# Attention's first stretch: where the scores of the block three later stand in a step of TensorE

## The reference, cut to what matters

```python
def _attn_ref(q, k, v, tau):
    scale = 1.0 / np.sqrt(q.shape[-1])
    scores = scale * np.matmul(q, k.transpose(0, 1, 3, 2))
    thresh = np.max(scores, axis=-1, keepdims=True) - tau
    scores = np.where(scores >= thresh, scores, -1000000000.0)
    scores = scores - np.max(scores, axis=-1, keepdims=True)
    attn = np.exp(scores)
    attn = attn / (np.sum(attn, axis=-1, keepdims=True) + 1e-09)
    return np.matmul(attn, v).astype(np.float32)
```

## Time and profile before

| | |
|---|---|
| Median of three runs | 1185.02 us (1183.88 to 1187.9) |
| The profiled execution's own time | 1193.75 us |
| Its span, from the first to the last instruction | 1192.0 us |
| PE busy | 1093.7 us, 92% of the span |
| DVE, ACT, POOL busy | 593.7, 439.3 and 347.3 us |
| Mean granted clock of PE | 0.953 |
| Last copy of a turned block in the first stretch ends | 112.8 us after the span's start |

### The profile page before, as it was taken

One profiled execution on the slowest core, in us unless ns is written; L12 is line 12 of the kernel. 1 busy time (PEld: TensorE's weight loads), 2 busy tenths in 40 slices (PEclk: granted clock), 3 DMA queues, 4 the chain that ended last, 5 costly groups with the idle time before them and its releaser, 6 DMA issues. The chain is left out here.

```text
span 1192.0 us, 20141 instructions
## 1 busy us (share of the span) xinstructions
PE 1093.7 (92%) x7130; PEld 956.7 (80%) x7131; DVE 593.7 (50%) x1164; ACT 439.3 (37%) x730; POOL 347.3 (29%) x324
## 2 busy tenths in 40 slices
PE   6889899999989999998999989899947999999995
PEld 5566699898979989887998987799946887887784
DVE  4565555656455565645556552222257344255641
ACT  5465443333354333335333332211144244144530
POOL 4454005433411452341235314055011121121111
PEclk9898999999999999989999988999957999999998
DMA  6776115335161452415134112022057335154501
GB/s 152 177 188 156 30 27 140 96 94 141 53 152 42 125 130 81 120 60 145 41 105 113 69 36 94 18 72 71 1 198 267 123 123 186 37 189 143 206 32 37
DMA packets 110650, 127.28 MB, mean 107 GB/s; under 512 B 67213, under 2 KB 67213, under 8 KB 110544
## 3 DMA queue, kind: packets, MB, share of 16 engines
q1 hardware_dynamic: 104480, 114.54, 33.9%
q0 software_dynamic: 3520, 10.75, 2.8%
q10 hardware_dynamic: 2544, 0.59, 0.2%
HBM read 87.90 MB, written 10.22 MB: 82 GB/s over the span
## 5 line engine op out<-in xcount | busy, mean ns | idle before, releaser
L753 ACT ACTIVATE ex<-score_banks,stat 128x576 f32<-128x576 f32 x132 | 97.8, 741 | 199.6 <-DVE stat L857 199.6
L657 PE MATMUL mlp_banks<-u_hi,w_hi 128*128 128x320 f32 (+1 forms) x512 | 159.2, 311 | 12.4 <-DVE hid_lo L916 9.5
L665 PE MATMUL mlp_banks<-hid_hi,w_hi 128*128 128x320 f32 (+1 forms) x512 | 158.7, 310 | 7.6 <-DVE z L924 7.2
L462 POOL TENSOR_TENSOR w_lo<-stage,w_hi 128x1024 fp32r<-128x1024 f32 x64 | 152.5, 2383 | 4.6
L657 PE MATMUL mlp_banks<-u_hi,w_lo 128*128 128x320 f32 (+1 forms) x512 | 153.1, 299 | 0.0
L657 PE MATMUL mlp_banks<-u_lo,w_hi 128*128 128x320 f32 (+1 forms) x512 | 153.1, 299 | 0.0
L665 PE MATMUL mlp_banks<-hid_hi,w_lo 128*128 128x320 f32 (+1 forms) x512 | 152.5, 298 | 0.0
L665 PE MATMUL mlp_banks<-hid_lo,w_hi 128*128 128x320 f32 (+1 forms) x512 | 152.4, 298 | 0.0
L458 POOL CAST w_hi<-stage 128x1024 fp32r<-128x1024 f32 x64 | 66.5, 1039 | 273.7 <-PE mlp_banks L657 233.1
L867 DVE SCALAR_TENSOR_TENSOR ex<-score_banks,stat,ex 128x576 f32<-128x576 f32 x132 | 107.9, 817 | 58.2 <-ACT ex L753 50.2
L857 DVE TENSOR_REDUCE stat<-score_banks 128x1 f32<-128x576 f32 x132 | 99.4, 753 | 39.7 <-PE score_banks L590 30.3
(11 more groups left out here) (228 smaller groups left out, 2046.4 us busy)
## 6 DMA issues: line engine op xcount, KB each, us to landing
stage<-in_moe_w_ch SPq DMA_DIRECT2D x64, 512.0 KB, 3.9
w_raw<-in_moe_w SPq DMA_DIRECT2D x64, 512.0 KB, 5.4
q_tiles<-q_parts SPq DMA_DIRECT2D x30, 320.0 KB, 4.1
q_tiles<-q_parts SPq DMA_DIRECT2D x60, 160.0 KB, 4.3
k_tiles<-k_parts SPq DMA_DIRECT2D x60, 144.0 KB, 3.5
raw_q<-in_q SPq DMA_DIRECT2D x32, 128.0 KB, 3.0
raw_v<-in_v SPq DMA_DIRECT2D x32, 128.0 KB, 2.9
raw_k<-in_k SPq DMA_DIRECT2D x28, 128.0 KB, 2.9
```

Source lines behind the costliest of these rows:

```text
L462: nc.gpsimd.tensor_tensor(w_lo[:, n % RING], stage[:, n % 2], w_hi[:, n % RING].bitcast(F32), ALU.subtract).then_inc(w_split, 1)
L657: last = nc.tensor.matmul(bank[:, 0:w], ch1(a, g, d, c), of[:, d, cols], start=(d == 0 and n == 0), stop=(d == KC - 1 and n == 2))
L665: last = nc.tensor.matmul(bank[:, 0:w], ch2(a, g, q, c), of[:, q, 0:w], start=(q == 0 and n == 0), stop=(q == QUARTER - 1 and n == 2))
L753: nc.scalar.activation(ex_of(n), score_of(n), ACT.Exp, bias=stat[:, n % 4, 0:1], scale=-1.0).then_inc(exp_done, 1)
```

## The change

In the loop over the first 36 steps, the wait for ACT's copy of block n and the scores of block n + 3 stand right behind the turn of block n. The parts of value products, raw turns and output turns of that step come after them.

```diff
         for n in range(ALONE):
             p, j, _, _ = place(n)
             turn(n)
+            if n + QUEUED < ALONE + 2:
+                pe.wait_ge(et_copied, n + 1)
+                scores(n + QUEUED)
             if p and j < 3:
                 values(p - 1, 1, ((0, 1), (2, 3), (4,))[j])
...
             if j == 7:
                 turn_out(p, 0)
-            if n + QUEUED < ALONE + 2:
-                pe.wait_ge(et_copied, n + 1)
-                scores(n + QUEUED)
```

## The result

| | before | after |
|---|---|---|
| Median | 1184.62 us (4 runs, 1183.88 to 1187.9) | 1221.23 us (4 runs, 1216.62 to 1228.15) |
| The profiled execution's own time | 1193.75 us | 1216.62 us |
| Its span | 1192.0 us | 1214.9 us |
| First turn to the last copy of the first stretch | 15.9 to 112.8 us: 96.9 us | 15.4 to 144.6 us: 129.2 us |
| Of it at the granted clock 0.50 | 13.7 us | 27.3 us |

The change makes the kernel slower: the ratio after to before is 1.0303, with a 95% interval of 1.025 to 1.0356, and the medians lie 36.6 us apart. 1222.4 us was predicted, in a range of 1202 to 1242.

A forecast was written before the change was run, and what follows sets the result against it. The prediction took PE, busy 92% of the span, as the bound. To the 1185.0 us median it added 18.7 us at full clock and 18.7 us for clock falls, giving 1222.4 us, range 1202 to 1242 us.

The forecast's parts named there:

- The wait loses its cover: Steps j = 0, 1, 4, 5, 6: PE waits uncovered for ACT's copy before scores, 0.86 us more each, 4.3 us a pair.
- Steps 3 and 7: Later output turns delay DVE's write and mask, hence the next turn: steps of 4.08 and 3.85 us, +1.5 and +1.3 us.
- Step j = 2: The same 0.86 us of uncovered copy, less a 0.33 us wait that goes: +0.5 us.
- The sum at full clock: First stretch, four pairs together: 4.0 + 1.1 + 7.1 + 6.5 = +18.7 us.
- the first pair: First pair of the stretch: steps 0 and 1 unchanged, later steps longer, step 8 freed of half clock; sum +4.0 us.
- The second pair's wait: PE's 2.85 us wait behind POOL's late weight transfer vanishes as PE comes later; the pair costs +1.1 instead of +7.6 us.
- The clock: First stretch: clock falls at seven places, mostly around steps 3 and 7, 6.8 us each; 48 us at half clock, +18.7 us.
- The low end of the term: Low bound of the loss from clock falls in the first stretch: 0, described as no more falls than before.
- rival A: The clock holds in the first stretch, leaving only the full-clock loss: 1204 us; chance 0.15.
- The sum: Whole kernel: 18.7 us at full clock plus 18.7 us from the clock, 37.4 us in total.

The follow-up runs named there:

- short_front: Changed kernel with ACT copying only the first of five 128-column pieces of turned blocks 0 to 7; first stretch 115.0 us, whole time not comparable.
- short_back: Kernel before with ACT copying only the first of five 128-column pieces of turned blocks 0 to 7; first stretch 93.1 us, whole time not comparable.
- half_cover: Changed kernel with each part of eight value products cut in two, four of them back between turn and scores; median 1205.6 us, ratio 1.0155.
- only_turn_outs: Kernel before with scores moved in front only in steps j = 3 and 7; median 1197.9 us, ratio 1.0099.
- fill_front: Changed kernel with five transposes of the identity added behind each turn to keep PE busy; median 1209.3 us, ratio 1.0181.
- queue_order: Kernel before with SP's starting transfers reordered, the third pair's q stacked ahead of V, U, two weight pieces and fourth pair's q and k; 1180.2 us.
- late_split: Kernel before with POOL's split of the first two weight pieces three steps later; median 1188.1 us, ratio 1.0019.
- queue_front: The transfer order of queue_order with the change's order on PE; median 1229.3 us, ratio 1.0347 to the kernel before.

## Why the prediction was right

**The wait loses its cover: right, a little too small.** 0.86 us a step was forecast; 0.93 to 1.12 was measured (3.44 and 3.52 us for j = 0 and 1, 3.29, 3.83 and 3.36 for j = 4, 5, 6). The pause itself was exact, 0.79 us, and PE's waits for the copies grew by 20.8 us in the stretch where some 20 were forecast. What was missed are the switches around the value products: they begin 0.72 us behind the scores (44.48, 45.20) where I took 0.63, and a turn that comes behind them takes 0.77 us instead of 0.71 until the copy can start. short_front and short_back show that the copy's length is what is paid, half_cover that four value products cover most of it.

**Steps 3 and 7: right.** 4.08 and 3.85 us were forecast, 4.07 and 3.80 measured, with the wait for DVE's mask of 1.0 and 1.25 us. only_turn_outs shows it by itself. Step j = 2 came to 3.25 us, +0.76 where I had +0.5, for the same switches.

**The sum at full clock.** A pair takes 30.8 us at full clock (fill_front: 104.96 - 74.19 = 30.77) where 29.8 was forecast, and queue_order's undisturbed pair 22.2. Over the stretch that is 119.2 - 88.6 = 30.6 us. Of it the disturbances of the kernel before, 8.3 us, go off: +22.3 where the prediction had +18.7. The term was mis-sized by the switches, 1.0 us a pair, and by the first pair, which came to 27.6 us, +4.6 instead of +4.0.

**The second pair's wait: right that the delay covers it, wrong that it is one transfer.** Two transfers come late in a row, the weight and the stacked q (late_split). PE's delay covered both: the turn of j = 5 in the second pair, which late_split could not begin before 56.29, comes at 62.54 in the changed kernel, with no wait for the mask.

**The clock: right in kind, too large.** Seven places with 6.8 us each were forecast, 48 us at half clock and 18.7 us of loss. The profiled execution has three, of 6.8, 10.2 and 10.2 us, 27.3 us in all: fewer than forecast, and longer. Their price is 10.0 us (129.2 - 119.2), 0.37 us for each us at half clock, which agrees with the 0.39 worked out. So of the three numbers it is the count of the places that failed most; the length of a fall was 9.1 us on average instead of 6.8.

Pauses like those around j = 3 and 7 make a fall possible, not certain. In the changed kernel j = 3 had a fall behind it in the second pair and none in the third, j = 7 in the third and none in the fourth, with the same pauses. queue_front, with the same order on PE, also had three of the seven, but others: j = 7 of the first and j = 3 and 7 of the fourth pair. The count was taken from one execution of the kernel before, with falls behind three of its four pairs; late_split and queue_order have the same pauses around steps 7 and 8 and no fall behind them, and that execution's mean clock, 0.953, is under those of all 46 later ones of the same kernel (0.955 to 0.966). What decides whether a given pause brings a fall stays open. The low end of the term, 0, was called "no more falls than before"; as the pairs in the sum were already freed of the falls of before, it stands for none at all. That is rival A, and fill_front shows what it would have given: +22.3 us, some 1207 us.

The Trainium skill, "TensorE: Matmul & The Clock Gate", states in "HAM oscillation — how this bites in real kernels" that one long idle gap is needed; no pause in the stretch is longer than 1.25 us, the clock fell three times, and it stopped falling when the pauses were filled. The measurement decides against that rule here, and agrees with the section "A second HAM failure mode: psum-queue depth-cycling".

**The sum.** 22.3 + 10.0 = 32.3 us in the stretch, against 37.4 forecast for the whole. The last copy came at 144.6 us where some 150 was forecast, with 27.3 us at half clock where it was 45. That the medians lie 36.6 us apart, so near to the forecast, is in good part luck: one term was 3.6 us too small and the other 8.7 us too large, and the medians lie 4.3 us further apart than the stretches of the two profiled executions. The changed kernel's executions spread over 11.5 us at mean clocks from 0.946 to 0.958, the slowest at the lowest; fill_front's spread over 3.5 us. With only two levels, the mean clock gives an execution's time at half clock, twice (1 - clock) times the span: 102, 109, 120 and 132 us for the four of the changed kernel, about 92 us at the 0.961 that is the median of the kernel before. So at the medians the two lie some 22 us of half clock apart, in the profiled stretches 13.6 (27.3 - 13.7); at 0.37 us each the other 9 us are an estimated 3 of the 4.3. Where in the program they lie was not seen.

## What to carry to other kernels

On an engine that works in order, a wait belongs behind whatever work doesn't need it: look for the work that stands between a producer and the wait for its consumer's answer before moving anything forward, and price the move by the latency that loses its cover, times the steps. Then follow each item that was moved back: a two-matmul output turn that feeds another engine's queue ahead of the next mask cost more per step than the uncovered copy alone. And where a transfer comes late, ask which one is next in the same queue; deferring the first only hands the wait to the second, while reordering the queue removed both.

## What was not expected of the hardware

Pauses of 0.79 to 1.25 us, repeated every three or four us, were enough for the clock to fall, in some places and not in others like them, and the falls lasted longer (6.8, 10.2 and 10.2 us) than the 3.4 us of two of the three before, behind which PE had no pause. Five transposes of the identity in each pause, work that nothing reads, made the changed kernel 12 us faster.
